# All of each chunk's regrouping by way of memory, in four writes and one read

## The reference

```python
def _attn_ref(q, kv, w_sr):                      # q (2, 12288, 128), kv (2, 384, 32, 128)
    kv_pool = kv.reshape(B, H // 4, 4, W // 4, 4, C).mean(axis=(2, 4))
    k = v = kv_pool.reshape(B, -1, C) @ w_sr     # 768 keys
    s = 1.0 / np.sqrt(C) * (q @ k.transpose(0, 2, 1))
    s = s - s.max(-1, keepdims=True)
    a = np.exp(s)
    a /= a.sum(-1, keepdims=True) + 1e-09
    return a @ v

x = attn_out.reshape(B * S, D)                   # 24576 x 128
h = x @ w1_in;  x = (h * np.cos(h)) @ w1_out     # d_ff 2048
h = x @ w2_in;  y = (h / (1 + np.exp(-1.702 * h))) @ w2_out
```

## Time and profile before

| what | value |
|---|---|
| median of 3 runs | 2722.08 us (2720.36 to 2723.69) |
| profiled execution, its own time | 2719.56 us |
| its span, first to last instruction | 2717.8 us |
| TensorE busy | 2612.0 us (96%) |
| VectorE / ScalarE / GpSimd busy | 2123.6 / 1918.6 / 2127.5 us |
| regrouping DMAs | 768, each 96 KB |
| moved by DMA in all | 156.15 MB |

### The profile page before, as it was taken

How to read it: one execution, slowest core, us unless ns; L and a number is a source line. 1 busy time by engine, 2 the same in 40 slices (tenths; PEclk the granted TensorE clock), 3 DMA queues, 4 the chain that set the end, 5 groups by cost and what they waited for, 6 DMA issues and landing times.

```text
span 2717.8 us, 37776 instructions
## 1 busy us (share of the span) xinstructions
PE 2612.0 (96%) x11797; PEld 2144.9 (79%) x11797; DVE 2123.6 (78%) x2264; ACT 1918.6 (71%) x2278; POOL 2127.5 (78%) x1784
## 2 busy tenths in 40 slices
PE   7888887888999999999999999999999999999999
PEld 6777666666888888888888888888888888888887
DVE  7777787878777787878787778787878787877776
ACT  4666676667777777777777777777777777777776
POOL 2555676767988888888888888888888888888883
PEclk9999999999999999999999999999999999999999
DMA  6877667661010000000000100000000000101000
GB/s 209 209 197 201 174 180 198 179 179 45 12 24 12 23 18 16 23 12 23 12 23 12 23 23 12 23 12 23 12 23 13 21 23 12 23 12 23 12 16 12
DMA packets 188842, 156.15 MB, mean 57 GB/s; under 512 B 117296, under 2 KB 142192, under 8 KB 187760
## 3 DMA queue, kind: packets, MB, share of 16 engines
q1 hardware_dynamic: 187728, 155.30, 21.9%
q10 hardware_dynamic: 1056, 0.13, 0.0%
HBM read 54.59 MB, written 25.26 MB: 29 GB/s over the span
## 4 chain that ended last, share of the span: by engine, by line
PE 78%; SPq 14%; DVE 2%; issue 2%; POOL 1%; ACT 1%; DMA 1%; DVEq 0%; POOLq 0%
PE psum L642 26%; PE psum L644 26%; PE psum L643 26%; SPq L442 12%; DMA gathered<-turned 1%; POOL g_lo L627 1%; DVE neg_max L1200 1%; ACT probs_t_hi L1000 1%; DVE turned L1212 1%; PE psum L714 1%; SPq L451 0%; ACT probs L989 0%; SPq L429 0%; PE psum L716 0%; SPq L456 0%
## 5 line engine op out<-in xcount | busy, mean ns | idle before, releaser
L627 POOL TENSOR_TENSOR g_lo<-g,g_hi 128x512 fp32r<-128x512 f32 x768 | 1134.0, 1477 | 65.6 <-ACT g_hi L1115 5.5
L1334 DVE TENSOR_TENSOR g_lo<-g,g_hi 128x1024 fp32r<-128x1024 f32 (+1 forms) x396 | 645.1, 1630 | 436.3 <-ACT g L1110 434.6
L1108 ACT ACTIVATE g_hi<-psum 128x1024 fp32r<-128x1024 f32 (+1 forms) x396 | 397.3, 1003 | 559.6 <-PE psum L644 559.5
L624 POOL CAST g_hi<-g 128x512 fp32r<-128x512 f32 x750 | 550.9, 735 | 234.3 <-DVE g L1325 234.3
L642 PE MATMUL psum<-g_hi,w_lo 128*128 128x512 f32 x1536 | 597.9, 389 | 0.8 <-POOL g_lo L627 0.8
L642 PE MATMUL psum<-x_hi,w_lo 128*128 128x512 f32 x1536 | 598.0, 389 | 0.0
L643 PE MATMUL psum<-x_lo,w_hi 128*128 128x512 f32 x1536 | 597.6, 389 | 0.0
L644 PE MATMUL psum<-x_hi,w_hi 128*128 128x512 f32 x1536 | 597.5, 389 | 0.0
L643 PE MATMUL psum<-g_lo,w_hi 128*128 128x512 f32 x1536 | 597.5, 389 | 0.0
L644 PE MATMUL psum<-g_hi,w_hi 128*128 128x512 f32 x1536 | 597.5, 389 | 0.0
L565 POOL TENSOR_TENSOR probs_t_lo<-gathered,probs_t_hi 128x1024 fp32r<-128x1024 f32 x140 | 334.6, 2398 | 226.4 <-ACT probs_t_hi L1000 226.3
(11 more groups left out here) (84 smaller groups left out, 2544.0 us busy)
## 6 DMA issues: line engine op xcount, KB each, us to landing
gathered<-turned SPq DMA_DIRECT2D x768, 96.0 KB, 2.2
x_dram<-x_out SPq DMA_DIRECT2D x48, 256.0 KB, 2.1
x_raw<-x_dram SPq DMA_DIRECT2D x48, 256.0 KB, 2.7
x_inv<-inverse_dram SPq DMA_DIRECT2D x48, 256.0 KB, 3.4
out<-y_blocks SPq DMA_DIRECT2D x190, 64.0 KB, 2.7
q_blocks<-in_q SPq DMA_DIRECT2D x47, 256.0 KB, 3.0
kv_all<-in_kv SPq DMA_DIRECT2D x6, 1024.0 KB, 9.6
kv_all<-in_kv SPq DMA_DIRECT2D x12, 512.0 KB, 6.3
```

The lines of the kernel that those rows point to most:

```text
L624: nc.gpsimd.tensor_copy(g1_hi[at][:, t], g1[at][:, t]).then_inc(g1_hi_ready, 1)
L627: nc.gpsimd.tensor_tensor(g1_lo[at][:, t], g1[at][:, t], g1_hi[at][:, t].bitcast(F32), ALU.subtract).then_inc(g1_lo_ready, 1)
L1108: nc.scalar.activation(g2_hi[ring2(j, p)][:, t], h2[buffer2(j)][:, t], ACT.Silu, scale=GELU)
L1334: nc.vector.tensor_tensor(g2_lo[ring2(j, p)][:, t], g2[ring2(j, p)][:, t], g2_hi[ring2(j, p)][:, t].bitcast(F32), ALU.subtract).then_inc(g ...
```

## The change

The sixteen SBUF-to-SBUF DMAs of a chunk become five by way of a tensor `bounce` in memory: for each group a of 32 partitions one write of 384 KB, whose 12 KB row of a partition is put down in four runs of 3 KB, one for each f; then, after SP has waited until all four writes have landed, one read of 1.5 MB, 128 partitions x 12 KB, into `gathered`. With `DIRECT = 0` the loop that still issues SBUF-to-SBUF DMAs runs over nothing.

The rest: ScalarE instead of VectorE adds 1e-9 to the totals; VectorE takes the reciprocal before the transpose (of 128x4) and copies the transposed 4x128 from PSUM; GpSimd instead of ScalarE rounds the last of the three parts, in all chunks but the last two; the last chunk's lower sums, the last x1 store and the last roundings move by a step or more.

```diff
-    REGROUPED = GROUPS * GROUPS * 16
+    DIRECT = 0
+    REGROUPED = (DIRECT * GROUPS + 1) * 16
+    BOUNCED = (GROUPS - DIRECT) * 16
+    BY_POOL = PARTS - 1
...
+    bounce = nc.dram_tensor("bounce", (CHUNKS, GROUPS, BLK, GROUPS * KEYS), F32,
+                            kind="Internal").ap()
...
+    def upper_made(engine, c, i):
+
+        if i == BY_POOL and c < CHUNKS - 2:
+            engine.wait_ge(probs_hi_by_pool, c + 1)
+        else:
+            engine.wait_ge(probs_hi_ready,
+                           c * BY_POOL + i + 1 + (PARTS - BY_POOL if c == CHUNKS - 1 else 0))
...
-                for a in range(GROUPS):
+                dst, src = gathered[b][c % 3], turned[b][n]
+                for a in range(DIRECT, GROUPS):
+                    at = slice((a - DIRECT) * KEYS, (a - DIRECT + 1) * KEYS)
+                    sp.dma_start(
+                        bounce[c][:, :, at].rearrange("f p x -> p f x"),
+                        src[a * BLK:(a + 1) * BLK, :, :, :].rearrange("p f k t -> p f (k t)")
+                    ).then_inc(bounced[n], 16)
+                for a in range(DIRECT):
                     for f in range(GROUPS):
-                        sp.dma_start(
-                            flat(gathered[b][c % 3][f * BLK:(f + 1) * BLK, a]),
-                            flat(turned[b][n][a * BLK:(a + 1) * BLK, f])
-                        ).then_inc(regrouped[n], 16)
+                        sp.dma_start(flat(dst[f * BLK:(f + 1) * BLK, a]),
+                                     flat(src[a * BLK:(a + 1) * BLK, f])
+                                     ).then_inc(regrouped[n], 16)
+                sp.wait_ge(bounced[n], BOUNCED * (c // 2 + 1))
+                sp.dma_start(dst[:, DIRECT:GROUPS].rearrange("p a k t -> p (a k t)"),
+                             bounce[c].rearrange("f p x -> (f p) x")
+                             ).then_inc(regrouped[n], 16)
...
+            def round_probabilities(c):
+
+                t = part_tiles(BY_POOL)
+                pool.wait_ge(regrouped[c % 2], REGROUPED * (c // 2 + 1))
+                if c >= 2:
+                    pool.wait_ge(values_summed, c - 1)
+                nc.gpsimd.tensor_copy(upper_part(c, BY_POOL),
+                                      gathered[c // CB][c % 3][:, :, t, :]
+                                      ).then_inc(probs_hi_by_pool, 1)
...
                 c, i = divmod(s - VALUES_SLOT, SUB)
+                if i == 0:
+                    round_probabilities(c)
...
-                pe.wait_ge(total_guarded, c + 1)
+                pe.wait_ge(total_inverted, c + 1)
...
+            up1(3, 3, 0)
             for i in range(PARTS):
                 sum_upper(CHUNKS - 1, i)
-            up1(3, 3, 0)
-            sum_lower(CHUNKS - 1, range(KT))
...
+                    if r * BODY + p == 4:
+                        sum_lower(CHUNKS - 1, range(KT))
...
+            def guard_totals(c):
+
+                cols = slice(c % 2 * SUB, (c % 2 + 1) * SUB)
+                act.wait_ge(exp_done, (c + 1) * SUB)
+                nc.scalar.activation(total[:, cols], total[:, cols], ACT.Copy,
+                                     bias=1e-9).then_inc(total_guarded, 1)
...
-                if c >= 0 and i < PARTS:
+                if c >= 0 and i < (BY_POOL if c < CHUNKS - 2 else PARTS):
                     round_probabilities(c, i)
+                if s % SUB == 1:
+                    guard_totals(s // SUB)
...
-                if static and r * BODY + p == 4:
+                if static and r * BODY + p == 5:
                     act.wait_ge(x1_ready, CHUNKS - 1)
                     store_x1(CHUNKS - 1)
...
-                if static and r * BODY + p == 1:
+                if static and r * BODY + p == 2:
                     for i in range(PARTS):
                         round_probabilities(CHUNKS - 1, i)
...
-            def guard_totals(c):
+            def invert_totals(c):
 
                 cols = slice(c % 2 * SUB, (c % 2 + 1) * SUB)
-                dve.wait_ge(exp_done, (c + 1) * SUB)
-                nc.vector.tensor_scalar(total[:, cols], total[:, cols], 1e-9, None,
-                                        ALU.add).then_inc(total_guarded, 1)
-
-            def invert_totals(c):
+                dve.wait_ge(total_guarded, c + 1)
+                nc.vector.reciprocal(total[:, cols], total[:, cols]).then_inc(total_inverted, 1)
+
+            def copy_inverses(c):
...
-                nc.vector.reciprocal(inverse[c % 2][:, :], total_ps).then_inc(inverse_ready, 1)
+                nc.vector.tensor_copy(inverse[c % 2][:, :], total_ps).then_inc(inverse_ready, 1)
```

More of the change, by code:

```diff
@@ L312, in attention_and_networks @@
     total_guarded = sem("total_guarded")
+    total_inverted = sem("total_inverted")
     total_turned = sem("total_turned")
@@ L315, in attention_and_networks @@
     turned_made = sem("turned_made")
+    bounced = [sem(f"bounced{n}") for n in range(2)]
     regrouped = [sem(f"regrouped{n}") for n in range(2)]
     probs_hi_ready = sem("probs_hi_ready")
+    probs_hi_by_pool = sem("probs_hi_by_pool")
     probs_lo_ready = sem("probs_lo_ready")
@@ L563, in lower_probabilities @@
                 b, t = c // CB, part_tiles(i)
-                pool.wait_ge(probs_hi_ready, c * PARTS + i + 1)
+                upper_made(pool, c, i)
                 nc.gpsimd.tensor_tensor(probs_t_lo[b][c % 3][:, :, t, :],
@@ L711, in sum_upper @@
                         pe.wait_ge(x1_ready, c - 1)
-                pe.wait_ge(probs_hi_ready, c * PARTS + i + 1)
+                upper_made(pe, c, i)
                 for t in range(KT)[part_tiles(i)]:
@@ L1242, in lower_probabilities @@
                 b, t = c // CB, part_tiles(i)
-                dve.wait_ge(probs_hi_ready, c * PARTS + i + 1)
+                upper_made(dve, c, i)
                 nc.vector.tensor_tensor(probs_t_lo[b][c % 3][:, :, t, :],
@@ L1295, in _ @@
                 if s % SUB == 2:
-                    guard_totals(s // SUB)
+                    invert_totals(s // SUB)
                 if s % SUB == 1 and s > SUB:
-                    invert_totals(s // SUB - 1)
+                    copy_inverses(s // SUB - 1)
                 if s - 1 in KEY_SLOTS:
@@ L1302, in _ @@
                     split_x1(0, 0)
-            invert_totals(CHUNKS - 1)
+            copy_inverses(CHUNKS - 1)
             def reduce_angle(i, p):
@@ L1390, in _ @@
                     store_x1(CHUNKS - 2)
+                if static and r * BODY + p == 2:
                     lower_probabilities(*LAST_LO[1])
-                if static and r * BODY + p == 2:
+                if static and r * BODY + p == 3:
                     lower_probabilities(*LAST_LO[2])
```

## The result

The changed kernel takes 2813.26 us (median of 4 runs, 2811.29 to 2818.95) against 2721.22 for the kernel before on the same chip: ratio 1.0339, 95% interval 1.0327 to 1.0351. The forecast was 2813. The number is right; as the experiments and the trace show, three of the terms that it was added up from are not, and their errors cancelled.

The account below looks back on a forecast made before the run. SP's queue, issuing sixteen DMAs a chunk, was taken as the bound at 12.16 us. Writes 6.6, read 3.7, other data 2.15 and gap 1.7 sum to 14.15, +94 us over 47 chunks: 2813 us, own range 2789 to 2881.

Parts of the forecast that it names:

- What bounded before, and SP's relief: Attention stage: SP's issue of sixteen DMAs sets 12.16 us a chunk; SP's own work falls from 11.5 to about 4.3.
- The period, 14.15 us: DMA time of one attention chunk, summed from data and gap: 14.15 us against 12.16 before, +94 us over 47 chunks.
- The writes, 6.6 us: Four writes of 32-partition slices to memory: today's regrouping price kept, 6.6 us a chunk; 8.3 by the skill page's figure.
- The read, 3.7 us: One read of 128 rows of 12 KB into `gathered`: 3.7 us a chunk at kv's 423 GB/s.
- The gap, 1.7: Between the last write's data and the read's start, none of this queue's DMAs in flight: 1.7 us, range 1.4 to 2.0.
- The loop through `turned`: VectorE's transpose of chunk c+2 waits for c's regrouping: 26 us for two chunks, 13 each, below 14.15, adds nothing.
- Share of 0.88: Sign of being right: the DMA engines' busy share in the attention stage rises from 0.71 to about 0.88.
- The other signs: Right: six us or more from last write's issue to read's, VectorE's and ScalarE's waits up; wrong: writes landing within 5 us.
- The edits on VectorE, ScalarE and GpSimd at nothing: Moved addition, reciprocal and rounding are covered by the DMA period; uncovered, worth up to 1 us a chunk.
- The clock: Rival, chance 0.09: TensorE's clock also falls after stalls, 1.2 us each, 56 us over 47 chunks: 2870.
- The end, within 3 us: After the last chunk's regrouping: 13.8 us against 11.56 + 2.1 before, counted as nothing, within 3 us.
- writes at full rate: Rival, chance 0.22: the receiving side halves today's rate, so writes take 3.7 us, period 11.25, 35 us faster: 2684.

Follow-up runs that it names:

- e1: The changed kernel with VectorE's first transpose of chunk c+2 waiting for chunk c's four writes instead of its read: 2792.68 us, ratio 1.0255.
- e5: The kernel before with all the change's other edits, but the sixteen copies within SBUF kept: 2723.38 us, ratio 1.000.
- e2: The changed kernel with one write of 128 partitions in 12 KB runs for the four writes, regrouping itself left out: 2787.25 us, ratio 1.0236.
- e12: The changed kernel with the read asked for in runs of 4 KB instead of 12 KB, same order and bytes: 2814.21 us, ratio 1.0335.

## Why the prediction was right, and where it was not

- **What bounded before, and SP's relief:** right. SP's queue went from 14% of the chain to 3%. "Nothing of issue on the chain" was a little too strong.
- **The period, 14.15 us:** measured 14.04 over the stage. By the records of single packets, in the mean of chunks 12 to 45, it is made up otherwise than forecast:

| term, us a chunk | forecast | measured |
|---|---|---|
| writes, data | 6.6 | 4.5 |
| read, data | 3.7 | 5.1 |
| stores, queries, weights, data | 2.15 | 2.1 |
| DMA engines without data | 1.7 | 2.4 |
| sum | 14.15 | 14.1 |

In order of time it is 5.80 us from the first byte written to the last, 1.34 to the first byte read, 6.15 to the last byte read, and 0.81 until the next write. The 0.81 is no waiting: the engines are busy for 0.78 of it, and more than half of it falls on the three chunks that load weights. The engines are without data for the whole of the 1.34, for some 0.6 in all while the writes start and run out, and for 0.3 in the read. The first twelve chunks were forecast near 15; they took (203.3 - 33.14)/12 = 14.2, where 203.3 is the start of the thirteenth chunk's writes.
- **The writes, 6.6 us:** too high by 2.1. This step took today's price over because source, slice and run length stay. The packets of 3 KB, 24576 in the whole run, have a median of 121 ns, against 211 ns for the same 24576 in the kernel before. So reading the slices did not by itself halve the rate. That the receiving side made the old copies slow fits this, but was not tried by itself. The Trainium skill (SBUF — State Buffer, Door 1: The DMA port swizzle) gives some 218 GB/s as the limit for partitions 0 to 31. Here four slices, which together cover all 128 partitions, were issued one behind the other and moved 395 GB/s in the window above; no run wrote one slice alone, so the limit for one was not tried. The forecast's estimate of 8.3 us for the writes, from that page's 189 GB/s, was not met: 5.8.
- **The read, 3.7 us:** too low by 1.4. The packets of 12 KB have a median of 496 ns and a 95th percentile of 1078. It goes with what runs beside: of chunks 12 to 43 (the later ones load no queries) the 16 reads that were followed by the query load within 3 us have 5.5 us of data (5.2 at least), the other 16 have 4.7 (5.0 at most). Why even these are above 3.7 is open.
- **The gap, 1.7:** 1.34 between the last byte written and the first byte read; the share of each of its three overheads wasn't tried. What the term left out is the time in which some of the engines are done and others not.
- **The loop through `turned`, "adds nothing":** wrong, and worth 21 us by e1. It was priced at 26 for two chunks and compared with 28.3; but SP's wait for the query transposes, which stands behind the same compute, was not in it. The sum and the loop came out alike (28.1 measured for two chunks), so the number held. In e1 the period of chunks 12 to 45 is 13.6 instead of 14.1: the writes' data falls from 4.5 to 4.0, since they are issued in time, the time without data from 2.4 to 2.1, and the read's data rises from 5.1 to 5.4.
- **Share of 0.88:** 0.82 measured. It rose from 0.71, as forecast, but less, because there is less data than summed and more time without it.
- **The other signs:** from the last write's issue to the read's it is 8.0 us in the mean, six or more in 45 of 48 chunks, as forecast, and no chunk's writes landed within 5 us of the first issue. VectorE's wait grew by tens of microseconds, ScalarE's did not: GpSimd's came in its place.
- **The edits on VectorE, ScalarE and GpSimd at nothing:** right, by e5 (1.000). The new 128x4 reciprocal takes 0.135 us, the copy 0.27, ScalarE's addition 0.19, GpSimd's rounding 1.04 against 1.5 forecast.
- **The clock:** it did fall, 0.97 to 0.88, and raising it again won nothing.
- **The end, within 3 us:** +3.3.
- **Two rows read too simply:** the window 85 to 90 us holds 15 packets of 4 KB beside the regrouping, which changes little. And "every transfer with memory on one side" at 365 to 423 GB/s leaves out the query load of the earlier trace rows, 0.48/(3.5 x 0.473) = 290.

The rival "writes at full rate" was to turn at writes of 4.6 us; their data was 4.5 in the mean, and its time still did not come, for it rested on the same 3.7 us of read and on a gap of 1.7. And e2, one write of all partitions, stayed at 1.0236. Writes 2.1 too high, read 1.4 and time without data 0.7 too low: the direction and the train on one queue were foreseen, but that the number met the measured one to the microsecond is luck.

## What to carry to other kernels

Five DMAs for sixteen were no gain here, where the five depend on each other: a write, a landing and a read in series are a train on one queue, and everything behind SP's wait joins it. Free each buffer on the transfer that really reads it, not on the end of the whole exchange; here that was worth 21 us. With half of the data on either way as well, +3.4% turned into -1.4%. And check a sum by its parts after the run, since here three wrong terms made a right total.

## What the runs showed of the hardware

Four writes of 32-partition slices to memory ran at 395 GB/s in one chunk and 277 in the next, with the same shapes and order: at the higher rate where all four were issued before the first byte moved. Copies of such slices within SBUF had 220 to 245. A read of 128 rows of 12 KB from memory, alone in its window, moved 340 GB/s where 8 KB rows had moved 423; in the mean of chunks 12 to 45 it had 5.1 us of data, 308 GB/s. From the last byte of the writes to the first byte of a read that waits for them it was 1.34 us. Spreading the rows from 12 to 13 KB won 10 us in 48 chunks. And in e12 a read written as three contiguous runs of 4 KB a row still moved in packets of 12 KB.
